# MLP tasks dealt to the attention's steps by weight, and x turned by true transposes under g times V

## The reference

```python
# attention, 4 batches, 8 heads, 576 tokens, 64 wide
scores = scale * np.matmul(q, k.transpose(0, 1, 3, 2))
thresh = np.max(scores, axis=-1, keepdims=True) - tau
scores = np.where(scores >= thresh, scores, -1000000000.0)
attn = softmax(scores)
x = (attn @ v) laid out as (4, 576, 512)
# MLP over tokens and channels
xt = x.transpose(0, 2, 1)
h = xt @ U @ V                                 # rank 32, the token mix
u = x + h.transpose(0, 2, 1)
x = u + np.maximum(u @ w_ch1, 0.0) @ w_ch2     # 512 -> 2048 -> 512
# experts: each row goes to one of 8, chosen by logits and a local gate
h = np.maximum(x[b, s] @ w1[e], 0.0)
out[b, s] = p[e] * (h @ w2[e])
```

## Time and profile before

| | us |
|---|---|
| median of 3 runs | 1145.09 (1145.08 to 1146.52) |
| the profiled execution | 1144.81 |
| its span | 1143.0 |
| busy PE / DVE / ACT / POOL | 1060.0 / 521.7 / 471.1 / 349.9 |

### The profile page before, as it was taken

How to read it: one execution, slowest core, us unless ns; L and a number is a source line. 1 busy time by engine, 2 the same in 40 slices (tenths; PEclk the granted TensorE clock), 3 DMA queues, 4 the chain that set the end, 5 groups by cost and what they waited for, 6 DMA issues and landing times. The chain is left out here.

```text
span 1143.0 us, 19941 instructions
## 1 busy us (share of the span) xinstructions
PE 1060.0 (93%) x7054; PEld 922.7 (81%) x7055; DVE 521.7 (46%) x1008; ACT 471.1 (41%) x894; POOL 349.9 (31%) x332
## 2 busy tenths in 40 slices
PE   6998999999789999979999998999759999999995
PEld 5765889999579999957999986999647887787784
DVE  4665544544354454434444542222385533245631
ACT  5775534444454444355444433111233533334630
POOL 4455122543303354330434431452120111111121
PEclk9999999999999999999999998999859999999998
DMA  7886051624335262442415212120256443155511
GB/s 160 192 184 179 19 135 48 162 72 122 123 70 115 68 162 73 124 128 63 114 49 141 74 38 79 47 87 15 96 188 247 144 148 115 58 180 180 180 38 34
DMA packets 110649, 127.26 MB, mean 111 GB/s; under 512 B 67213, under 2 KB 67213, under 8 KB 110544
## 3 DMA queue, kind: packets, MB, share of 16 engines
q1 hardware_dynamic: 104480, 114.54, 35.3%
q0 software_dynamic: 3520, 10.75, 2.9%
q10 hardware_dynamic: 2544, 0.59, 0.2%
HBM read 87.90 MB, written 10.22 MB: 86 GB/s over the span
## 5 line engine op out<-in xcount | busy, mean ns | idle before, releaser
L783 ACT ACTIVATE ex<-score_banks,stat 128x576 f32<-128x576 f32 x132 | 97.9, 741 | 183.0 <-DVE stat L920 183.0
L473 POOL CAST w_hi<-stage 128x1024 fp32r<-128x1024 f32 x64 | 66.6, 1041 | 305.8 <-PE mlp_banks L682 260.4
L682 PE MATMUL mlp_banks<-u_hi,w_hi 128*128 128x320 f32 (+1 forms) x512 | 157.0, 307 | 3.1 <-ACT u_hi L833 2.3
L690 PE MATMUL mlp_banks<-hid_hi,w_hi 128*128 128x320 f32 (+1 forms) x512 | 158.1, 309 | 0.8 <-DVE hid_lo L969 0.8
L929 DVE SCALAR_TENSOR_TENSOR ex<-score_banks,stat,ex 128x576 f32<-128x576 f32 x132 | 107.7, 816 | 108.7 <-ACT stat L787 107.1
L478 POOL TENSOR_TENSOR w_lo<-stage,w_hi 128x1024 fp32r<-128x1024 f32 (+1 forms) x70 | 154.1, 2204 | 4.8
L682 PE MATMUL mlp_banks<-u_hi,w_lo 128*128 128x320 f32 (+1 forms) x512 | 151.4, 296 | 0.0
L690 PE MATMUL mlp_banks<-hid_hi,w_lo 128*128 128x320 f32 (+1 forms) x512 | 151.3, 296 | 0.0
L682 PE MATMUL mlp_banks<-u_lo,w_hi 128*128 128x320 f32 (+1 forms) x512 | 151.3, 296 | 0.0
L690 PE MATMUL mlp_banks<-hid_lo,w_hi 128*128 128x320 f32 (+1 forms) x512 | 151.3, 295 | 0.0
L920 DVE TENSOR_REDUCE stat<-score_banks 128x1 f32<-128x576 f32 x132 | 99.4, 753 | 35.8 <-PE score_banks L615 26.9
(11 more groups left out here) (233 smaller groups left out, 1975.0 us busy)
## 6 DMA issues: line engine op xcount, KB each, us to landing
stage<-in_moe_w_ch SPq DMA_DIRECT2D x64, 512.0 KB, 3.6
w_raw<-in_moe_w SPq DMA_DIRECT2D x64, 512.0 KB, 5.5
q_tiles<-q_parts SPq DMA_DIRECT2D x30, 320.0 KB, 4.4
q_tiles<-q_parts SPq DMA_DIRECT2D x60, 160.0 KB, 4.3
k_tiles<-k_parts SPq DMA_DIRECT2D x60, 144.0 KB, 3.5
raw_q<-in_q SPq DMA_DIRECT2D x32, 128.0 KB, 3.2
raw_v<-in_v SPq DMA_DIRECT2D x32, 128.0 KB, 2.7
raw_k<-in_k SPq DMA_DIRECT2D x28, 128.0 KB, 2.7
```

Of the source, the lines that this page charges most:

```text
L473: nc.gpsimd.tensor_copy(w_hi[:, n % RING], stage[:, n % 2]).then_inc(w_upper, 1)
L682: last = nc.tensor.matmul(bank[:, 0:w], ch1(a, g, d, c), of[:, d, cols], start=(d == 0 and n == 0), stop=(d == KC - 1 and n == 2))
L690: last = nc.tensor.matmul(bank[:, 0:w], ch2(a, g, q, c), of[:, q, 0:w], start=(q == 0 and n == 0), stop=(q == QUARTER - 1 and n == 2))
L783: nc.scalar.activation(ex_of(n), score_of(n), ACT.Exp, bias=stat[:, n % 4, 0:1], scale=-1.0).then_inc(exp_done, 1)
```

## The change

`tasks_by_step` no longer takes a fixed number of tasks per step (two, or three at `j` 6 and 8). Each kind of task has a weight in `WEIGHT`, each place of an attention step one in `ATTENTION`, and from the third step of a batch (the second for batch 1) each step takes tasks as long as the sum of both stays under an equal share. The two last tasks of a batch's MLP (`LATE`) and one gate go into the next batch's first step. In a `mixed` task the blocks of x are turned by transposes that come first, and g times V is added onto them.

```diff
+LATE = 2
...
+WEIGHT = {"token_mix": 10240, "mixed": 2048, "hidden": 3 * KC, "channel": 3 * QUARTER, "gate": 512, "logits": 512, "rows": 1024}
+ATTENTION = [11000, 4300, 3200, 2700, 9000, 3200, 2700, 4000, 2700]
+def weight(t):
+    kind, k, *_ = TASKS[t % NTASK]
+    return WEIGHT[kind] * (WIDTH[k] if kind in ("hidden", "channel") else 1)
...
-        ready = NTASK * b - (TAIL if at < ALONE else 0)
-        if b == 1 and at < 2:
-            want = at
-        elif at < 2:
-            ready = NTASK * (b - 1)
-            want = 4 if at == 0 else TAIL
-        elif at == 2:
-            want = 1
+        first = 2 if b > 1 else 1
+        if at < first:
+            take = 0 if b == 1 else LATE + 1 if at == 0 else NTASK * (b - 1) - done
         else:
-            want = 3 if j in (6, 8) else 2
-        if n == NBLK - 1 or at == ALONE - 1:
-            want = PER_GROUP
-        take = max(0, min(want, ready - done))
+            end = NTASK * b - TAIL - (LATE if b < B - 1 else 0)
+            if at == first:
+                rest = sum(weight(t) for t in range(done, end)) + sum(ATTENTION[i % STEPS] for i in range(first, ALONE))
+                share, used = rest / (ALONE - first), 0
+            used += ATTENTION[at % STEPS]
+            take = 0
+            while done + take < end and (at == ALONE - 1 or used + weight(done + take) / 2 < share * (at - first + 1)):
+                used += weight(done + take)
+                take += 1
...
-                nc.tensor.matmul(bank[:, 0:w], g4[:, c * P:(c + 1) * P], v4[:, START[k]:START[k] + w], start=True, stop=True)
                 for n, i in enumerate(range(*BLOCKS[k])):
-                    last = nc.tensor.matmul(bank[:, n * P:n * P + ROWS[i]], x[:, i, c * P:(c + 1) * P], ident[:, 0:ROWS[i]],
-                                            start=False, stop=True, skip_group_check=True)
+                    nc.tensor.matmul(bank[:, n * P:n * P + ROWS[i]], x[0:ROWS[i], i, c * P:(c + 1) * P], ident[0:ROWS[i], 0:ROWS[i]], is_transpose=True,
+                                     start=(n == 0), stop=False, skip_group_check=True)
+                last = nc.tensor.matmul(bank[:, 0:w], g4[:, c * P:(c + 1) * P], v4[:, START[k]:START[k] + w], start=False, stop=True, skip_group_check=True)
```

More of the change, by code:

```diff
@@ L84, in tasks_by_step @@
         b, at = divmod(n, ALONE)
-        j = at % STEPS
         if b == 0:
```

## The result

The kernel with the change takes 1164.65 us (median; 1159.65 to 1166.3) against 1145.8 us of the kernel before in the same session: ratio 1.0151, 95% interval 1.0119 to 1.0183, or 17.3 us (13.6 to 21.0) on 1145. The forecast was 1155.0 with a range to 1162.0: right in sign, too small by 7.1 us going by the ratio (by 9.7 between 1155.0 and the median), and outside its range. The profiled execution took 1166.3 us with a granted clock of 0.967 over the span. The other three took 1159.65 us at 0.974, and 1163.94 and 1165.36 us at 0.968. The prediction named a clock under 0.97 as a sign of being wrong, and three of the four runs show it.

What follows compares the result with a forecast made beforehand. The prediction took PE's issued work to bound the middle of a batch. 22.4 us lost less 4.8 + 5.7 + 1.7 = 12.2 won gave 10.2 us slower, 1155 us, range 1148 to 1162.

Steps and rivals of the forecast that it cites:

- a clock under 0.97: Granted clock over the whole span; the prediction named a value below 0.97 as a sign of being wrong.
- bare turns: 20 mid-batch steps with no task behind the scores' turn: PE waits for ACT's copy, 1.12 us each, 22.4 us lost.
- turns of batches: Where one batch gives way to the next: 4.8 us won at steps 71, 107, 143, and 5.7 by mixed tasks.
- the transposes: In mixed tasks, transposes replace matmuls that turn x, 80 matmuls fewer; 1.7 us won in the last batch.
- What bounds the kernel: Mid-batch, time is the sum of what PE issues; moving tasks between steps wins nothing there by itself.
- packing of the mixed tasks: At the starts of batches' MLPs, mixed tasks go into three steps in place of four or five: 5.7 us won.
- covered ends: Steps 71, 107 and 143 get two tasks, so their turns are covered: 2.7, 1.1 and 1.0, sum 4.8 us won.
- gates and logits: In steps 73 and 109 they precede the row tasks; set at nothing (bounds 0.9 won, 1.5 lost in each).
- one chain, from step 76 to 78: Second batch's mixed tasks: step 78 starts at 326.7 in place of 328.7, 2.0 us won.
- The clock falls: Rival: stretches at 1.2 GHz also in batches 2 and 3, longer in the last; 5 to 8 us more, 1161; chance 0.2.
- Both sides cancel: Rival: bare turns cost 15.8 us, turns of batches give 3.6 us more than found; 1145; chance 0.07.
- the copy stays hidden: Rival: ACT's copy causes no wait at bare turns, so only what is won counts; 1133; chance 0.07.

Runs made afterwards that it cites:

- table_alone: The change with the mixed tasks of the kernel before (no transposes): 1161.53 us, ratio 1.0122 to the kernel before.
- deal_covered: The change with the old mixed tasks, at least one task in each middle step, a single hidden or channel task behind the turn: 1140.76 us, ratio 0.9970.
- bare_turns: The kernel before, with surplus tasks moved one step on at the 20 steps the prediction names: 1168.89 us, ratio 1.0205.
- covered_ends: The kernel before, with tasks moved within a batch so that steps 71, 107 and 143 have two each: 1141.26 us, ratio 0.9975.
- change_covered: The change with at least one task in each middle step, a single hidden or channel task behind the turn: 1145.25 us, ratio 1.0006.
- packed_mixed: `covered_ends` with the change's numbers of tasks in steps 38 to 42, 75 to 78 and 111 to 114: 1141.03 us, ratio 0.9960.
- turns_alone: The kernel before with the change's mixed tasks (transposes first): 1151.40 us, ratio 1.0048.
- turns_twice: The kernel before with the change's mixed tasks, each transpose made twice: 1148.44 us, ratio 1.0028.
- mixed_twice: `covered_ends` with all matmuls of a mixed task made twice over in its bank, 192 more: 1146.09 us, ratio 1.0004.
- change_covered_twice: `change_covered` with each transpose of a mixed task made twice: 1149.16 us, ratio 1.0029.
- turns_full: The kernel before with the change's mixed tasks, the third block of 64 rows turned as a full 128: 1148.15 us, ratio 1.0040.

## Why the prediction was wrong

The terms, forecast and measured (us, by ratios on 1145):

| step | forecast | measured | from |
|---|---|---|---|
| bare turns | +22.4 | +17.4 | table_alone less deal_covered; 23.5 in bare_turns alone |
| turns of batches | -10.5 | -3.4 | deal_covered |
| the transposes | -1.7 | +3.3 | change less table_alone; 4.1 and 5.5 on other deals |
| sum | +10.2 | +17.3 | the change |

The rows add up because each is a difference of two kernels in the list. Against the forecast the turns of batches give 7.1 us less and the transposes 5.0 less, together 12.1, and the bare turns cost 5.0 less, which leaves the 7.1 by which the sum is off.

**What bounds the kernel.** Right. The middle of a batch is what PE issues: moving tasks there changed little but the covers, and the deal with all turns covered came out level with `covered_ends` (0.6 us apart).

**Bare turns.** Right in mechanism, place and size: 0.79 us of wait at each of the 20 steps named. The price of 1.12 us is confirmed alone (22.7 to 23.5 us for 20). Within the change's deal it is 0.87 by the ratios (17.4 / 20). The traces give it without the scatter of clock and experts. From the turn of step 44 to that of 71, from 81 to 107 and from 117 to 143 the clock is 1.00 and the same tasks pass; `table_alone` takes 19.8 us longer there than `deal_covered` (7.6, 6.4 and 5.7), and the change 19.9 longer than `change_covered`: 0.99 for each turn, 0.79 of it idle, inside the bounds of 15.8 and 22.4. So of the 5.0 us in the table 2.6 are a turn that was priced 0.13 too high, and the rest is within the uncertainty of the ratios (2.7). Why a turn costs less in this deal than in `bare_turns` stays open.

**Turns of batches.** This step failed, and its largest part was the packing of the mixed tasks. The covered ends were priced at 4.8 and gave 2.9 to 3.6 over all runs (5.0 up to the end of the last MLP, in the profiled executions). The gates and logits at nothing was right for the waits (2.79 us against 2.78). The packing was priced at 5.7 and gave 0.2 to 1.7. The prediction worked out one chain, from step 76 to 78, and let the first and third batch follow it. It saw the wait of the third mixed task for its bank and put it inside a net gain; `packed_mixed` shows that the mixed tasks' waits (11.2 us over the run, from 2.2) take back the whole of what the scores no longer wait, so that of the 5.7 us 1.5 are saved as idle time. These went to matmuls at 1.2 GHz, for which the chain worked out had no term. The work that has to pass through ACT, DVE and two banks was the same, only in fewer steps.

**The transposes.** This step failed in sign. The arithmetic of PE was right for a task of 256 tokens: g times V starts 0.17 us after two transposes, and the next mixed task 0.37 us after the first (719.73 to 720.10) where it took 0.56, and the last batch's eight came down, to the first hidden matmul behind them, from 10.87 us to 9.94:

```profile
719.73 0.41 PE L681 MATMUL mlp_banks<-ident,x 128*128 128x128 f32 x2 [2.02 <-DVE hid_hi L972]
719.90 0.36 PE L683 MATMUL mlp_banks<-v,hid_hi 128*128 128x256 f32 x1
720.10 0.38 PE L681 MATMUL mlp_banks<-ident,x 128*128 128x128 f32 x2
...
729.67 0.55 PE L692 MATMUL mlp_banks<-u_hi,w_hi 128*128 128x256 f32 x1
```

The prediction had about 9 us for the eight. Two things were left out of the sum. The clock is one, which the prediction has only as a rival: that last matmul lasts 0.55 us in place of 0.36, and the hidden tasks behind it run at 1.2 GHz up to 735 us. The mean clock falls by 0.007 on both deals where it was tried on its own (`turns_alone`, `change_covered`). What that is worth is seen within one kernel: over 32 runs of the kernel before, a least-squares line gives 0.65 us for each 0.001 of clock. Seven thousandths are 4.6 us, against 4.1 and 5.5 measured. So as an estimate the transposes are worth about nothing at an equal clock, neither the 1.7 won nor a loss; with an uncertainty of 2 us and more in each figure, the 1.7 are not excluded. The other is the pause behind a transpose of 64 rows. The prediction took adding g times V onto the transposes to cost what it costs now; in a task of 320 tokens it starts 0.51 us after the first transpose, and three matmuls fewer save 0.06 us (0.83 to 0.77 from start to start), where 0.33 were counted.

**The rivals.** "The clock falls" (1161, chance 0.2) was the nearest, and in the profiled execution right about the second batch's start and the longer stretch in the last; the third batch kept its clock (1.00 from 480 to 550 us). Its price of 5 to 8 us is about what the transposes came out worse than forecast (5.0). It kept the gain of the packing, and its 1161 too lies below the 1164.65. "Both sides cancel" and "the copy stays hidden" fell with `bare_turns`. As a whole, the forecast booked 7.4 us (5.7 and 1.7) as won in the steps of mixed tasks, and in and just behind these the low clock fell.

**What stays open.** That the transposes lower the mean clock is shown on two deals. That the clock goes with the work PE has in the stretches of mixed tasks is argued: `turns_twice` and `mixed_twice` bear it out (both up) and `change_covered_twice` weakly (up), but `turns_full` rose with less busy time, and of three kernels with the same packing only `packed_mixed` fell. Why the clock of `change_covered_twice` varies from 0.966 to 0.979 from run to run was not found, so the loss to the clock is shown, and what would surely prevent it isn't.

## What to carry to other kernels

Where an order is written out by hand, count not the tasks in a step but what stands behind each producer whose copy the next instruction waits for; 20 missing covers of 1 us undid the whole deal, and three added ones were nearly all of its gain. Packing work through a chain of two banks hardly shortened it here (1.5 us of idle time where 5.7 us were counted): look where the wait goes before it is booked as won. And where PE is lightly filled, taking matmuls away from it can cost more in the clock of the full work behind than it saves; compare the granted clock before calling fewer instructions a gain.

## What the runs showed of the chip

- Work made twice can be free: on the old deal 80 added transposes brought the clock from 0.967 to 0.974, and the time did not rise (2.3 us less, uncertain by 2.7). With both edits and all turns covered they cost 2.6 us by the ratios (uncertain by 2.9) and 3.9 between the medians.
- The clock differs from run to run of one kernel (0.965 to 0.971 and 1142.43 to 1149.66 us in `change_covered`), and the spread follows it in part: over the 32 runs of the kernel before, the line on the clock explains about half of the variance.
- A transpose of a block of 64 rows, followed by a matmul of 128 rows, holds PE 0.27 us longer than one of 128 rows (g times V starts after 0.51 us in the change, 0.24 in `turns_full`).
- A result that ACT copies for the next matmul, with nothing behind its producer on PE, left PE idle for 0.79 us at each of 20 places, and cost 0.99 us each in the change's deal.
